# Attention in another order on all four engines of a fused attention, experts and gated kernel

## What is computed

```python
    scores = scale * np.matmul(q, k.transpose(0, 1, 3, 2))
    keep = is_sink | in_window
    scores = np.where(keep, scores, -1000000000.0)
    scores = scores - np.max(scores, axis=-1, keepdims=True)
    a = np.exp(scores)
    a = a / (np.sum(a, axis=-1, keepdims=True) + 1e-09)
    return np.matmul(a, v).astype(np.float32)
```

## Time and profile before

| | us |
|---|---|
| median of three runs | 375.54 (375.26 to 375.56) |
| the profiled execution | 375.04 |
| its span, first to last instruction | 373.2 |
| TensorE busy | 365.4 (98%) |
| VectorE busy | 213.5 (57%) |
| ScalarE busy | 191.8 (51%) |
| GpSimd busy | 143.1 (38%) |

### The profile page before, as it was taken

One profiled execution on the slowest core, in us unless ns is written; L12 is line 12 of the kernel. 1 busy time (PEld: TensorE's weight loads), 2 busy tenths in 40 slices (PEclk: granted clock), 3 DMA queues, 4 the chain that ended last, 5 costly groups with the idle time before them and its releaser, 6 DMA issues.

```text
span 373.2 us, 7754 instructions
## 1 busy us (share of the span) xinstructions
PE 365.4 (98%) x2854; PEld 334.4 (90%) x2854; DVE 213.5 (57%) x614; ACT 191.8 (51%) x512; POOL 143.1 (38%) x188
## 2 busy tenths in 40 slices
PE   7799999999999999999999999999999999999996
PEld 6577777789998889999988998899999988999996
DVE  3687777632588884068898618633745265325342
ACT  4888888854678782468888353332311033411110
POOL 4898888888746017100455617510000032100000
PEclk9999999999999999999999999999999999999999
DMA  8655555342330000000131201000011200000112
GB/s 251 207 179 189 182 166 180 95 139 83 109 93 2 2 2 2 2 0 3 38 106 35 96 28 56 2 0 2 0 43 44 85 2 0 0 2 0 45 41 85
DMA packets 12885, 24.20 MB, mean 65 GB/s; under 512 B 1328, under 2 KB 6704, under 8 KB 12848
## 3 DMA queue, kind: packets, MB, share of 16 engines
q1 hardware_dynamic: 12848, 23.70, 20.1%
HBM read 20.55 MB, written 3.15 MB: 63 GB/s over the span
## 4 chain that ended last, share of the span: by engine, by line
PE 92%; ACT 3%; POOL 2%; issue 2%; DVE 1%; DVEq 0%; ACTq 0%; POOLq 0%
PE banks L991 15%; PE banks L993 15%; PE banks L992 15%; PE banks L1250 14%; PE banks L1066 5%; PE banks L1034 5%; PE banks L1149 5%; PE banks L1017 5%; PE banks L1185 5%; PE banks L1161 4%; PE banks L1076 2%; ACT Pa L511 2%; POOL Pa L419 1%; PE banks L1004 1%; ACT Pb L577 1%
## 5 line engine op out<-in xcount | busy, mean ns | idle before, releaser
L511 ACT ACTIVATE Pa<-Pa,NMa 128x260 f32<-128x260 f32 (+1 forms) x96 | 46.1, 483 | 12.7 <-DVE NMa L697 12.7
L697 DVE CUSTOM_DVE_ANT_0 Pa<-banks,win 128x260 f32<-128x260 f32 (+1 forms) x96 | 33.6, 402 | 18.0 <-PE banks L1017 18.0
L419 POOL TENSOR_TENSOR Pa<-Pa,RIa 128x520 f32<-128x520 f32 (+1 forms) x48 | 42.3, 912 | 0.0
L492 POOL TENSOR_TENSOR rstd<-vare,minus_half 128x1 f32<-128x1 f32 x12 | 11.9, 990 | 77.6 <-DVE vare L926 77.6
L577 ACT ACTIVATE Pb<-Pb,NM 128x384 f32<-128x384 f32 (+5 forms) x48 | 31.8, 664 | 5.8 <-DVE NM L787 5.4
L677 ACT ACTIVATE gH<-uT 128x384 fp32r<-128x384 f32 x16 | 8.4, 525 | 49.9 <-DVE uT L945 49.9
L787 DVE CUSTOM_DVE_ANT_0 Pb<-banks,causal 128x384 f32<-128x384 f32 (+5 forms) x48 | 28.4, 620 | 7.7 <-PE banks L1149 5.5
L1250 PE MATMUL banks<-w_sgL,vnH 128*128 128x384 f32 x96 | 32.5, 338 | 0.0
L943 DVE TENSOR_TENSOR vb<-banks,b_all 128x384 f32<-128x384 f32 x16 | 8.9, 558 | 37.0 <-PE banks L1250 37.0
L1017 PE MATMUL banks<-kd,qd 64*128 64x260 f32 (+1 forms) x192 | 26.9, 392 | 1.2 <-DMA qd<-in_qT 1.2
L1034 PE MATMUL banks<-ident,Pa 128*128 128x128 f32 x176 | 25.0, 281 | 1.8 <-POOL Pa L419 1.6
(11 more groups left out here) (153 smaller groups left out, 1075.6 us busy)
## 6 DMA issues: line engine op xcount, KB each, us to landing
va<-in_v SPq DMA_DIRECT2D x8, 384.0 KB, 3.7
out<-raw SPq DMA_DIRECT2D x16, 192.0 KB, 1.9
kd<-in_kT SPq DMA_DIRECT2D x7, 396.0 KB, 3.4
qd<-in_qT SPq DMA_DIRECT2D x7, 384.0 KB, 4.4
vs<-in_vsink SPq DMA_DIRECT2D x8, 336.0 KB, 4.4
raw<-in_w_sgT SPq DMA_DIRECT2D x9, 256.0 KB, 2.7
raw<-in_w_in SPq DMA_DIRECT2D x8, 256.0 KB, 2.7
raw<-in_w_b SPq DMA_DIRECT2D x8, 193.0 KB, 4.7
```

Of the source, the lines that this page charges most:

```text
L419: nc.gpsimd.tensor_tensor(Pa[s][:, h, ts, :], Pa[s][:, h, ts, :], RIa[:, s, h, ts].unsqueeze(2).broadcast_to((P, ts.stop - ts.start, WIN)) ...
L511: nc.scalar.activation(Pa[s][:, h, t, a:WIN], Pa[s][:, h, t, a:WIN], ACT.Exp, bias=NMa[:, s, h, t:t + 1], scale=-1.0, accum_out=RSa[:, s, ...
L697: nc.vector.tensor_tensor_reduce(out=Pa[s][:, h, t, a:WIN], in0=banks[:, score_bank(p, t) + 2 * (t % 2) + h, 0:WIN - a], in1=m[:, :], scal ...
```

## The change

The loops are replaced by one list of steps for each engine (`A_PE`, `A_ACT`, `A_DVE`, `A_POOL`), a string for the first pair, one for the pairs behind it, and for TensorE two for the end. A token is a letter and numbers: `s` scores, masks or takes the exponential of a tile of the same pair, `n` of the next pair, `t` turns group g.h, `c` copies or scales it, `k` is the sinks' transpose, its copy or their gathering, `v` weighs a third (tiles 2g and 2g + 1) and `w` the sinks of the pair before, `x` takes or splits the pair before's result, `i` and `j` invert sums, `l` splits a strip, `r` projects. The last numbers of a TensorE token are its banks.

- Scores 4 and 2: in the middle pairs TensorE weighs a third of the pair before, scores four tiles of the next pair in one run (`n0 n5 n1 n2`), weighs the other two thirds, scores the last two tiles (`n4 n3`), adds the sinks, and then turns all six groups and the sinks in a run.
- Scores, groups and transposed sinks share the banks 0 to 5 in any order. A step waits for whoever read the bank last (`used_before`, `wait_bank_taken`).
- ScalarE copies four groups of a pair and VectorE two, in the first pair ScalarE two and VectorE four.
- The first pair's sums are inverted in three parts (`i1`, `i0`, `i2`), each for two tiles, and GpSimd scales a group as soon as its part is there.
- GpSimd splits the strip behind the pair's scaling and gathering, no longer ahead of it.
- The six later filler matmuls are gone. The mask of every tile waits for the turning and gathering of the pair that had the buffer, not only that of tile 0.
- The sink step of weighing waits for the copied sinks itself; before, the fourth tile of the weighing did.

```diff
-TURNS = [(0, 1, "dve"), (1, 1, "dve"), (0, 0, "act"), (1, 0, "act"), (2, 0, "dve"), (2, 1, "act")]
-TURN_N = len(TURNS)
-A_TURN, A_SUM = 4, 6
+TURN_N = 2 * GROUPS
+A_SUM = 6
...
+A_PE = [order("s0.0.1 s3.2.4 s2.5.3 s1.4.2 s4.1.0 n1.4.2 s5.0.5 n0.0.1 n3.2.4 n2.5.3 t1.0.2 n5.0.5 t1.1.4 n4.1.0 t0.0.3 t0.1.4 t2.0.5 k1 t2.1.0"),
+        order("v1 n0.2.1 n5.5.4 n1.3.0 n2.1.2 v2 v0 n4.3.0 n3.1.4 w t1.1.0 t1.0.4 t0.0.5 t0.1.3 t2.1.1 t2.0.2 k0"),
+        order("v1 v2 v0 w t1.1.4 t1.0.5 r0 t0.0.2 t0.1.3 r1 t2.1.4 t2.0.5 k3"),
+        order("r2 r3 v1 v2 v0 w")]
+A_ACT = [order("s0 s3 s2 s1 s4 s5 n1 n0 n2 n5 n4 n3 c0.0 c2.1"),
+         order("n0 n5 n2 n1 n4 x n3 c1.0 c0.0 c2.1 c0.1")]
+A_DVE = [order("s0 s3 s2 s1 s4 i1 n1 s5 i0 n0 n3 n2 i2 n5 c1.1 n4 c1.0 c0.1 c2.0 k j"),
+         order("n0 n5 n2 n1 n4 n3 c1.1 x j c2.0 k")]
+A_POOL = [order("c1.0 c1.1 c0.1 c0.0 c2.0 c2.1 k l"),
+          order("c0.0 c0.1 c1.0 c1.1 c2.1 c2.0 k l")]
...
+def in_pair(p, steps):
+
+    shift = {"n": 1, "j": 1, "v": -1, "w": -1, "x": -1}
+    steps = [(step[0], p + shift.get(step[0], 0), *step[1:]) for step in steps]
+    return [x for x in steps if 0 <= x[1] < PAIRS or x[0] == "r"]
+
+
+A_PE_STEPS = [x for p, steps in enumerate([A_PE[0]] + [A_PE[1]] * (PAIRS - 2) + A_PE[2:]) for x in in_pair(p, steps)]
+A_ACT_STEPS, A_DVE_STEPS, A_POOL_STEPS = [[x for p in range(PAIRS) for x in in_pair(p, steps[min(p, 1)])] for steps in (A_ACT, A_DVE, A_POOL)]
...
+def bank_uses(step):
+
+    if step[0] in "sn":
+        return [(bank, ("s", *step[1:3], h)) for h, bank in enumerate(step[3:])]
+    return [(step[-1], step[:-1])] if step[0] in "tk" else [(PROJ_BANKS[0][step[2]], step)] if step[0] == "r" else []
+
+
+A_USES = [use for step in A_PE_STEPS for use in bank_uses(step)]
...
+def used_before(use):
+
+    k = A_USES.index(use)
+    return ([None] + [what for bank, what in A_USES[:k] if bank == use[0]])[-1]
...
-                    sp.wait_ge(s_["scored"], T * (p - 1))
+                    sp.wait_ge(s_["scored"], max(A_SCORED[p - 2, t] for t in range(T)))
...
-            def scale_pair(p):
+            def scale_group(p, g, h):
 
                 s = p % 2
-                pool.wait_ge(s_["sums_inverted"], p + 1)
-                for g, h, _ in TURNS:
-                    if g == 0:
-                        nc.gpsimd.tensor_tensor(Pa[s][:, h, 0, P:WIN], Pa[s][:, h, 0, P:WIN], RIa[:, s, h, 0:1].broadcast_to((P, BLK)), ALU.mult)
-                    ts = slice(max(2 * g, 1), 2 * g + 2)
-                    nc.gpsimd.tensor_tensor(Pa[s][:, h, ts, :], Pa[s][:, h, ts, :],
-                                            RIa[:, s, h, ts].unsqueeze(2).broadcast_to((P, ts.stop - ts.start, WIN)), ALU.mult)\
-                        .then_inc(s_["scaled"], 1)
+                pool.wait_ge(s_["sums_inverted"], inverted(p, g))
+                if g == 0:
+                    nc.gpsimd.tensor_tensor(Pa[s][:, h, 0, P:WIN], Pa[s][:, h, 0, P:WIN], RIa[:, s, h, 0:1].broadcast_to((P, BLK)), ALU.mult)
+                ts = slice(max(2 * g, 1), 2 * g + 2)
+                nc.gpsimd.tensor_tensor(Pa[s][:, h, ts, :], Pa[s][:, h, ts, :],
+                                        RIa[:, s, h, ts].unsqueeze(2).broadcast_to((P, ts.stop - ts.start, WIN)), ALU.mult)\
+                    .then_inc(s_["scaled"], 1)
 
...
-            for p in range(PAIRS):
-                split_strip(p)
-                scale_pair(p)
-                gather_sinks(p)
+            for what, p, *at in A_POOL_STEPS:
+                if what == "l":
+                    split_strip(p)
+                elif what == "c":
+                    scale_group(p, *at)
+                else:
+                    gather_sinks(p)
...
-                if t == 0 and p >= 2:
+                if p >= 2:
                     dve.wait_ge(s_["turned"], TURN_N * (p - 1))
                     dve.wait_ge(s_["sinks_gathered"], p - 1)
-                dve.wait_ge(s_["scored"], T * p + t + 1)
+                dve.wait_ge(s_["scored"], A_SCORED[p, t])
...
+            def invert_sums(p, g=None):
 
                 s = p % 2
-                dve.wait_ge(s_["expd"], 2 * T * (p + 1))
-                nc.vector.tensor_scalar(RIa[:, s, :, :], RSa[:, s, :, :], EPS_SUM, None, ALU.add).then_inc(s_["dve_step"], 1)
-                dve.wait_ge(s_["dve_step"], p + 1)
-                nc.vector.reciprocal(RIa[:, s, :, :], RIa[:, s, :, :]).then_inc(s_["sums_inverted"], 1)
+                ts = slice(0, T) if g is None else slice(2 * g, 2 * g + 2)
+                dve.wait_ge(s_["expd"], 2 * max(A_EXPD[p, t] for t in range(T)[ts]))
+                nc.vector.tensor_scalar(RIa[:, s, :, ts], RSa[:, s, :, ts], EPS_SUM, None, ALU.add).then_inc(s_["dve_step"], 1)
+                dve.wait_ge(s_["dve_step"], inverted(p, g))
+                nc.vector.reciprocal(RIa[:, s, :, ts], RIa[:, s, :, ts]).then_inc(s_["sums_inverted"], 1)
...
+            def wait_bank_taken(use):
+
+                before = used_before(use)
+                if before is None:
+                    return
+                what, p, *at = before
+                if what == "s":
+                    t, h = at
+                    wait("masked", 2 * A_MASKED[p, t] - 1 + h)
+                elif what == "k":
+                    wait("sinks_in", p + 1)
+                else:
+                    for who, copied in A_COPIED.items():
+                        wait("turned_in_" + who, copied.get(before[1:], 0))
+
+            def score_tile(p, t, *at):
 
                 s = p % 2
-                if p == 0 and t == 0:
+                if p == 0 and t < 2:
                     pe.wait_ge(first_in, 32)
-                elif t == 0 or (p == 0 and t == 2):
+                else:
                     pe.wait_ge(qk_in[s], 32 * (p // 2 + 1))
-                wait("masked", masks_ahead(p, t))
                 c, w = (0, BLK) if t == 0 else ((t - 1) * BLK + SINK, WIN)
-                for h in range(2):
...
+            def turn_group(p, g, h, bank):
+
+                pe.wait_ge(s_["scaled"], A_SCALED[p, g, h])
+                wait_bank_taken((bank, ("t", p, g, h)))
...
+                pe.wait_ge(s_["sinks_in"], p + 1)
...
-                elif b == 0 and bank < 4:
-                    wait("masked", 2 * T * PAIRS)
+                elif b == 0 and n < EARLY_PROJ[0]:
+                    wait_bank_taken((bank, ("r", *[x[1] for x in A_PE_STEPS if x[0] == "r" and x[2] == n], n)))
                 elif b == 0 and bank < 6:
-                    wait("turned_in_act", GROUPS * PAIRS)
-                    wait("turned_in_dve", GROUPS * PAIRS)
+                    for who, copied in A_COPIED.items():
+                        wait("turned_in_" + who, max(copied.values()))
+                    wait("sinks_in", PAIRS)
```

More of the change, by code:

```diff
@@ new lines, with counted @@
+A_ACT_STEPS, A_DVE_STEPS, A_POOL_STEPS = [[x for p in range(PAIRS) for x in in_pair(p, steps[min(p, 1)])] for steps in (A_ACT, A_DVE, A_POOL)]
+def counted(steps, letters, keep=4):
+    return {x[1:keep]: n + 1 for n, x in enumerate([x for x in steps if x[0] in letters])}
+A_SCORED, A_MASKED, A_EXPD = [counted(x, "sn", 3) for x in (A_PE_STEPS, A_DVE_STEPS, A_ACT_STEPS)]
+A_TURNED, A_SCALED = counted(A_PE_STEPS, "t"), counted(A_POOL_STEPS, "c")
+A_COPIED = {"act": counted(A_ACT_STEPS, "c"), "dve": counted(A_DVE_STEPS, "c")}
@@ new lines, with inverted, score_banks @@
+A_INVERTED = counted(A_DVE_STEPS, "ij", 3)
+def inverted(p, g):
+    return A_INVERTED.get((p, g), A_INVERTED.get((p,)))
+def bank_uses(step):
[3 more added lines that the diff above has]
+A_USES = [use for step in A_PE_STEPS for use in bank_uses(step)]
+def score_banks(p, t):
+    return next(x[3:] for x in A_PE_STEPS if x[0] in "sn" and x[1:3] == (p, t))
@@ L115 @@
              [("kq", e, 1) for e in range(E)] + [("v", 4, 1), ("v", 5, 1), ("v", 3, 1)]
-WARM_UP, WARM_LATER = 9, 6
-def score_bank(p, t):
-    return 4 if (p, t // 2) in ((0, 1), (1, 0)) else 0
-def masks_ahead(p, t):
-    k = T * p + t
-    if k < 4:
-        return 0
-    return 2 * (k - 3 if k < 2 * T - 2 else k - 1)
-def copies_by(who, g):
-    return [sum(w == who for _, _, w in TURNS[:n + 1]) for n, (group, _, w) in enumerate(TURNS) if group == g and w == who]
+WARM_UP = 9
 MIXES = [(g, m) for g in range(2) for m in range(KT)]
@@ L1033, in turn_group @@
                         continue
-                    last = nc.tensor.transpose(banks[:, A_TURN + n % 2, j * P:(j + 1) * P], Pa[p % 2][:, h, t, own * BLK:own * BLK + P], ident[:, :])
+                    last = nc.tensor.transpose(banks[:, bank, j * P:(j + 1) * P], Pa[p % 2][:, h, t, own * BLK:own * BLK + P], ident[:, :])
                 last.then_inc(s_["turned"], 1)
```

167 lines of the change are left out of this document (60 added, 107 removed).

## The result

The changed kernel takes 381.14 us (median of four, 380.6 to 381.47) against 375.55 of the kernel before beside it (375.26 to 376.03): a ratio of 1.0146, 95% interval 1.0129 to 1.0164. It is 5.6 us slower; 374.7 was forecast. The profiled execution took 381.36 with a span of 379.6 (before 373.2), and its mean granted clock is 0.996.

What follows compares the result with a forecast made beforehand. TensorE's issue bounds the attention stage. Hand-over terms -1.63 - 0.11 + 0.83 = -0.9 took the profiled 375.04 to 374.1; the median, 0.5 higher, gave 374.6, with small delays 374.7 (range 373.7 to 376.3).

Steps and rivals of the forecast that it cites:

- Runs of TensorE, 9.00 a pair: Attention stage: two score runs a pair instead of four, so TensorE's pair falls from 9.55 to 9.00 us.
- Each small delay ... I take 0.8.: Whole kernel: delays left at nothing cost time once the 0.2 to 0.4 spare is used; gain 0.8, not 0.9.
- Do the others keep up?: Each pair: ScalarE 8.3 and GpSimd 8.2 of 9.0 us, VectorE gives a copy away; all fit, TensorE sets the pair.
- ScalarE closes the ring: Rival, chance 0.20: a release 0.1 longer makes the first score tile wait; pair 9.15 to 9.2, whole 375.5 us.
- Start: First pair: first scaling at 9.6 instead of 12.51, sinks' transpose at 16.3 instead of 19.03, 2.75 us earlier.
- Strip 7 and the gap: Hand-over: strip 7 behind pair 7's scaling; projection at 79.0 instead of 80.64, TensorE idle about 3.3 us before it.
- The last sinks' wait: Pair 7's sinks' transpose waits 0.8 us for ScalarE's copy of group 0.1, which stands behind 2.1.
- The clock: Rival, chance 0.14: the gap before the first projection slows TensorE's clock, costing 1.8 us; whole 376.5 us.
- What follows is TensorE-bound and moves as it is: Behind the last weighing: the rest of the program shifts with its start, its own length unchanged.

Runs made afterwards that it cites:

- e_best1: Kernel after with buffer waits on the first mask tile only and new orders in the first, steady and last pairs: 373.53 us, ratio 0.9954.
- e_steady_order: Kernel after with buffer waits on the first mask tile only and e_best1's orders in the six steady pairs alone: 380.03 us, ratio 1.012.
- e_short_exp: Kernel after with buffer waits on the first mask tile only and exponentials of tiles 3 and 4 over 128 of 260 columns: 378.17 us, ratio 1.0067.
- e_copy_to_dve: Kernel after with the copy of group 0.1 on VectorE instead of last on ScalarE: 380.14 us, ratio 1.0133.
- e_one_inversion: Kernel after with the first pair's sums inverted at once instead of by thirds: 383.13 us, ratio 1.0204.
- the 13 fillers: Kernel after with 13 filler matmuls on TensorE ahead of the first projection's wait for the strips: 379.46 us, ratio 1.011.
- e_strip_inside: Kernel after with strip 7 split on GpSimd ahead of the last pair's last two scalings instead of behind its gathering: 377.18 us, ratio 1.0056.
- the four kernels with the new steady orders: e_best1 (373.53 us), e_steady_order (380.03), and e_best1 with a third of the last weighing behind the fourth projection (373.57) or one VectorE step moved (374.0).

## Why the prediction was wrong, step by step

The prediction put the end of the last weighing 0.9 us earlier; it came 6.4 later. The 7.3 between are accounted for by these steps.

- **Runs of TensorE, 9.00 a pair.** The step that failed, 3.9 us over five pairs and 0.65 in the first. Three terms. The sum itself was 0.20 short: with no wait left the pair is 9.20 (e_best1, e_steady_order). All of it lies in the run of four score tiles. It takes 1.94 (46.32 to 48.26), where the rows of before make 1.72: the short and a full tile 0.86 (66.98 to 67.84) and two more at 0.43. The other runs come out as forecast: weighing 1.03 and 1.68, two score tiles 1.08, sinks 0.81, the 23 transposes with their switches 2.66. Why four tiles in a run cost more than their sum wasn't tested. The chain that closes through ScalarE's copy of group 1.0 and the places around it was another 0.25 (9.45 with the mask waits cured), of which e_short_exp frees 0.18. And the three waits on each mask tile were 0.34. Together 0.79 a pair, which is the measured 9.79.
- **"Each small delay ... I take 0.8."** The waits on the masks were in the diff, and the prediction gave small waits 0.1 us in all, out of a spare of 0.2 to 0.4 a pair. There was no spare. The 0.134 us ahead of a mask come back in the ring: 0.13 ahead of the second score run, 0.14 in the run of transposes, 0.34 a pair on the mean. The kernel before, with the same waits, shows them at nothing.
- **Do the others keep up?** As loads, yes: ScalarE 8.65, GpSimd 8.19, VectorE 7.32 of 10. As a chain, no. The rival "ScalarE closes the ring" had the right kind of mechanism with too small a price (9.15 to 9.2), and its reason, the load, finds no support in e_copy_to_dve.
- **Start.** First scaling 10.20 instead of 9.6, and two waits of 0.32 for the thirds instead of one of 0.3: the transpose at 17.30, not 16.28. The mechanism stands, 1.7 to 2.0 us by e_one_inversion; its size was 1.0 too good. The idle stretches there (0.50, 0.53, 0.62, 0.78) were taken as covered. What the removed fillers did in this stretch wasn't tested.
- **Strip 7 and the gap.** Right: 3.07 us of idle time for 3.3, at the place and by the mechanism named. From the sinks' transpose of pair 6 to the projection 8.35 us, for 8.3.
- **The last sinks' wait.** Right: 0.72 for 0.8, by ScalarE's copy of group 0.1, and gone when VectorE makes that copy.
- **The clock.** A rival with 0.14 and +1.8; it happened, and costs 1.6 (14.11 against the forecast's 12.46 from the projection to the end of the weighing; 1.7 by the 13 fillers). The Trainium skill ("TensorE: Matmul & The Clock Gate", Part 1) says that the clock falls when the engine has stood idle and comes back after sustained work. The traces here agree: after 3.07 and 5.28 us of idle time it is at half, after 0.69, and after 0.66 and 0.53, it is not. At the start of e_strip_inside, though, it fell with no idle stretch above 0.84 us just ahead of it (last section).
- **What follows is TensorE-bound and moves as it is.** Right for the kernel after (280.8 in both), not for the four kernels with the new steady orders, which take 281.7 to 282.3 there.

The rivals were priced one at a time. Two of them, the ring and the clock, came true at once, and the small waits and the late start beside them, all on the slower side. Nothing in the range stood for their sum.

## What to carry to other kernels

When an edit takes spare time out of a ring of engines, price each wait in the diff again: an instruction that was free before can then be paid in each round. Read the ring as a chain from release to release, not as loads; an engine busy 8.65 of 10 can close it. And look first at the hand-over to the next stage: here it waited for one late step, a faster ring brought nothing (e_steady_order), and the idle stretch was paid a second time in the clock.
